# Reciprocals on VectorE as a Newton step on a ScalarE guess, with logarithms and exponentials in groups

## The chip, the cores and the metric

The kernel runs on one core of one Trainium2 chip. The metric is device time in microseconds (us) of that core; less is better.

## What is computed

Three stages in float32: a linear attention with a complex, data-dependent decay, then two feed-forward layers.

```
mag = sqrt(a_re**2 + a_im**2)
scale = minimum(mag, 0.999) / (mag + 1e-6);  a = a * scale        # per channel and token
for t in range(768):                       # S is complex, 48 x 48 per head
    S = a[t][:, None] * S + outer(k[t], v[t])
    y[t] = q[t] @ real(S)
h = y @ w_in                               # 3072 tokens, 384 -> 2048
x = (max(h, 0) + alpha * min(h, 0)) @ w_out
out = x + gate * relu(x @ w1[e]) @ w2[e]   # only tokens with x @ w_skip > 0; e = argmax(x @ w_gate)
```

Batch 4, 8 heads, 768 tokens, head size 48. The division by mag + 1e-6 is one of the two reciprocals of this document. The other comes from the way in which the recurrence is computed: a chunk of 128 tokens is done with matmuls, for which q is multiplied by the product F of the chunk's gates up to its token, and k by 1/F, that is by the conjugate of F over |F|**2. The kernel needs 1/|F|**2 for that.

## The kernel before, in words

Phase 1 works in eight halves of 384 tokens (3 chunks of 128) and runs three things beside each other. A step (`step(h, mlp_too, more)`, written once for each engine) does attention for half h, the first feed-forward layer for half h-1, and prepares the gates of half h+1. The first call (step 0) has no feed-forward layer, the last (step 7) has no next gates, and a last feed-forward layer follows alone. Six of the eight steps are in a loop of three rounds with two steps each. Phase 2 (the experts) comes after and isn't touched.

The order of every engine's work is written out by hand. Between the attention parts stand the blocks of the feed-forward layer, `of_mlp(f)`, f from 0 to 15, with a tail to 18 on TensorE and 16 on the others. For a block f TensorE computes h into `mlp_ps` (L513); ScalarE makes `bent`, a scaled relu of it (L652); VectorE joins it with h to `g` (L907, "the fused operation of f"); ScalarE copies the high part of g of the block before (L658, "high"); VectorE subtracts it to get the low part (L912, "low"); and TensorE uses the parts of block f-3 for the output (L523). `mlp_ps` has two buffers, so TensorE's block f waits for VectorE's fused operation of f-2.

The gates of the next half are prepared by these parts, per chunk of 384 columns:

- `square_gates` (ScalarE, L603), `sum_gates` (VectorE, L770), `root_gates` (ScalarE, L607), `pad_gates` (ScalarE, L613, adds 1e-6), `scale_gates` (VectorE: reciprocal L778, fused minimum and product L780, product L784);
- `within`, `across` and `carry` (VectorE): the running complex products of the gates in a chunk;
- `square_products` and `take_factors` (ScalarE, L626 and L622), `sum_products` (VectorE, L840), `inverse` (VectorE, reciprocal L847), `decay_qk` (VectorE: k times the inverse, L856, then q and k times F, L862).

`decay_qk(nxt, 0)` stands at the end of a step, `decay_qk(h, 1)` and `(h, 2)` in the middle of the next. SyncE's queue is in order too: after `decay_qk(nxt, 0)` it issues the ten moves of q and k to the layout of the heads (`move_qk`, L348), at the end of the step the stores of the finished rows (L380, L381), and at the start of the next the loads of the following half's gates (`load_gates`, L316). TensorE's `scores` of a chunk wait for its moves. `low_y` (L877) and `next_state` (L889 to L901) take a chunk's results out of PSUM on VectorE, `high_y` (L647) does on ScalarE, and `mask_scores` (L870) masks the scores of a chunk on VectorE.

```
sp.wait_ge(qk_made, made)                                 # move_qk: ten moves follow
sp.wait_ge(x2_taken, val(n.n * NC + 2 * NC))              # store_x2: two stores follow
pe.wait_ge(g_made, val(n.n * NF + f + 1))                 # up(n, f), g_made starts at 2
pe.wait_ge(g_lo, val(n.n * NF + f + 4))                   # down(n, f), g_lo starts at 3
act.wait_ge(g_made, val(n.n * NF + f + 3))                # high_g(n, f)
```

## Time and profile before

| | |
|---|---|
| median of 3 runs | 1044.0 us (1043.59 to 1044.29) |
| the profiled execution | 1042.54 us, its span 1040.8 us |
| granted TensorE clock, mean | 0.883 |
| TensorE busy (matmuls) | 765.3 us, 74% of the span |
| VectorE (DVE) busy | 731.2 us, 70% |
| ScalarE (ACT) busy | 320.6 us, 31% |
| GpSimd (POOL) busy | 106.9 us, 10% |
| reciprocals of `scale_gates`, L778 | 24, 61.1 us |
| reciprocals of `inverse`, L847 | 24, 60.0 us |
| phase 1 | to about 813.5 us |

The profile lists one execution. Busy time is the time in which an engine works on an instruction; L778 is line 778 of the kernel before. A share over the whole span mixes stages with different limits, so the prediction reads stretches of it. TensorE's granted clock is given as a share of full speed: its two levels are 1.2 and 2.4 GHz, and a mean between them is a mix.

### The profile page before, as it was taken

To read this page: it belongs to the slowest core of one execution; us is meant where nothing else is said; L and a number is where in the kernel's file an instruction comes from. 1 tells how busy PE (TensorE), PEld (TensorE's weight loads), DVE (VectorE), ACT (ScalarE), POOL (GpSimd) and SP (SyncE) were. 2 spreads that over 40 slices of the span, in tenths; PEclk is the share of its full clock that TensorE was granted. 3 is DMA by queue.
4 is the path that set the end of the run, shared out by engine and by line. 5 is a ranking of instruction groups with operands and counts; after the bars stand their busy time and mean duration, and the time that the engine had idled before them with its cause. 6 is when DMAs were issued, how large, how long until landed. Compare 5 with 4: busy or idle time off the path is not lost. (4 is left out here: it accounts for less than half of the span.)

```text
span 1040.8 us, 16040 instructions
## 1 busy us (share of the span) xinstructions
PE 765.3 (74%) x5430; PEld 735.9 (71%) x5431; DVE 731.2 (70%) x1328; ACT 320.6 (31%) x613; POOL 106.9 (10%) x94
## 2 busy tenths in 40 slices
PE   1514529987896888789689778979999300989897
PEld 1514428877896888689588778869999200989896
DVE  6997988997997899799789979976433410343343
ACT  5532114334232423423242342233333210232321
POOL 4610000000000000000000000000000064232232
PEclk9998668997997898899889989989999755899899
DMA  6633324215233421523342152333210591144440
GB/s 191 211 92 90 101 55 139 53 45 160 66 83 92 121 65 46 164 64 81 94 127 58 45 168 58 82 95 93 61 52 1 211 319 9 34 149 143 146 149 16
DMA packets 87585, 104.82 MB, mean 101 GB/s; under 512 B 21142, under 2 KB 73536, under 8 KB 87488
## 3 DMA queue, kind: packets, MB, share of 16 engines
q1 hardware_dynamic: 84928, 99.76, 32.8%
q0 software_dynamic: 2560, 3.78, 1.2%
q8 instruction: 60, 0.98, 0.4%
q14 instruction: 37, 0.30, 0.1%
HBM read 61.07 MB, written 12.25 MB: 70 GB/s over the span
## 5 line engine op out<-in xcount | busy, mean ns | idle before, releaser
L523 PE MATMUL out_ps<-w_out_hi,g_parts 128*128 128x394 f32 x768 | 235.7, 365 | 36.8 <-DVE g_parts L912 36.8
L513 PE MATMUL mlp_ps<-xT,w_in_hi 128*128 128x384 f32 x768 | 218.0, 367 | 16.7 <-DMA xT<-y_parts 8.1
L523 PEld LDWEIGHTS out_ps<-w_out_hi,g_parts 128*128 128x128 f32 x768 | 154.1, 204 | 42.0 <-DVE g_parts L912 42.0
L513 PEld LDWEIGHTS mlp_ps<-xT,w_in_hi 128*128 128x128 f32 x768 | 147.9, 205 | 21.7 <-issue 12.4
L523 PE MATMUL out_ps<-w_out_lo,g_parts 128*128 128x394 f32 x384 | 138.9, 362 | 0.0
L652 ACT ACTIVATE bent<-mlp_ps,bend_size 128x384 f32<-128x384 f32 x128 | 74.3, 580 | 207.3 <-PE mlp_ps L513 207.1
L513 PE MATMUL mlp_ps<-xT,w_in_lo 128*128 128x384 f32 x384 | 136.6, 356 | 0.0
L907 DVE SCALAR_TENSOR_TENSOR g<-mlp_ps,slope_side,bent 128x384 f32<-128x384 f32 x128 | 78.6, 615 | 79.6 <-ACT bent L652 69.9
L459 PE MATMUL att_ps<-kq 112*128 112x128 f32 x384 | 54.7, 302 | 58.4 <-DMA kq<-qk_dec 58.4
L459 PEld LDWEIGHTS att_ps<-kq 112*128 112x128 f32 x384 | 52.2, 215 | 61.0 <-DMA kq<-qk_dec 47.8
L1250 PE MATMUL mlp_ps<-xT_e,w_sb 128*128 128x128 f32 x624 | 82.3, 297 | 13.1 <-issue 11.5
L1250 PEld LDWEIGHTS mlp_ps<-xT_e,w_sb 128*128 128x128 f32 x624 | 80.5, 212 | 15.6 <-issue 14.2
L658 ACT ACTIVATE g_parts<-g 128x384 fp32r<-128x384 f32 x128 | 66.4, 518 | 59.3 <-DVE g L907 57.1
L523 PEld LDWEIGHTS out_ps<-w_out_lo,g_parts 128*128 128x128 f32 x384 | 78.5, 204 | 0.0
L513 PEld LDWEIGHTS mlp_ps<-xT,w_in_lo 128*128 128x128 f32 x384 | 78.5, 204 | 0.0
L1504 POOL IOTA e_index_i<- 128x8 int32 x1 | 0.1, 134 | 758.5 <-POOLq L135 758.5
L912 DVE TENSOR_TENSOR g_parts<-g,g_parts 128x384 fp32r<-128x384 f32 x128 | 70.1, 548 | 0.3
L1467 DVE SCALAR_TENSOR_TENSOR hT<-mlp_ps,hT 128x256 fp32r<-128x256 f32 x52 | 22.0, 424 | 68.9 <-ACT hT L1322 65.5
L778 DVE RECIPROCAL sq<-sq 128x384 f32<-128x384 f32 x24 | 61.1, 2544 | 1.3 <-ACT sq L613 1.3
L467 PE MATMUL att_ps<-ident,kq 112*128 112x112 f32 x192 | 30.8, 295 | 40.8 <-DVE probs L870 40.8
L847 DVE RECIPROCAL inv<-norms 128x384 f32<-128x384 f32 x24 | 60.0, 2527 | 0.0
L1264 PE MATMUL out_ps<-w_hi,hT 128*128 128x384 f32 x208 | 56.1, 340 | 0.0
(138 smaller groups left out, 1116.2 us busy)
## 6 DMA issues: line engine op xcount, KB each, us to landing
kq<-qk_dec SPq DMA_DIRECT2D x96, 144.0 KB, 3.1
w_sb<-in_w SPq DMA_DIRECT2D x8, 1536.0 KB, 7.3
w_raw<-in_w SPq DMA_DIRECT2D x8, 1536.0 KB, 11.8
gates<-in_a SPq DMA_DIRECT2D x24, 384.0 KB, 5.1
qk_raw<-in_qk SPq DMA_DIRECT2D x24, 384.0 KB, 3.2
xT<-y_parts SPq DMA_DIRECT2D x48, 144.0 KB, 2.8
v_nat<-in_v SPq DMA_DIRECT2D x24, 192.0 KB, 3.1
out<-x SPq DMA_DIRECT2D x8, 576.0 KB, 3.1
```

The source lines that it names most:

```text
L459: last = pe.matmul(ps[:, n * CH:(n + 1) * CH], kq[:, slot, 1, :], kq[:, slot, 0, :], start=True, stop=True)
L467: last = pe.transpose(ps[:, n * ROWS:(n + 1) * ROWS], kq[:, PAIRS * half + n, 1, :], ident[0:ROWS, 0:ROWS])
L513: last = pe.matmul(ps[:, 0:HT], w_in_v[s][:, kk, f * P:(f + 1) * P], xT[n.p][:, kk, m, :], start=(kk == 0 and j == 0), stop=(kk == KT - 1 ...
L523: last = pe.matmul(out_ps[i][:, 0:DL], g_parts[:, f % 4, s, i * P:(i + 1) * P], w_out_v[m][:, f, :], start=(f == 0 and j == 0), stop=(f == ...
L652: act.activation(bent[:, f % 2, :], mlp_ps[f % 2][:, 0:HT], ACT.Relu, scale=bend_size[:, f:f + 1]).then_inc(bent_made, 1)
L658: act.activation(g_parts[:, f % 4, 0, :], g[:, f % 3, :], ACT.Copy).then_inc(g_hi, 1)
L778: dve.reciprocal(s1, s0).then_inc(norm_inv, 1)
L847: dve.reciprocal(of_chunk(inv[:, :], c), of_chunk(norms[:, :], c)).then_inc(f_inverted, 1)
L907: dve.scalar_tensor_tensor(out=g[:, f % 3, :], in0=mlp_ps[f % 2][:, 0:HT], scalar=slope_side[:, f:f + 1], in1=bent[:, f % 2, :], op0=ALU.m ...
L912: dve.tensor_tensor(g_parts[:, f % 4, 1, :], g[:, f % 3, :], g_parts[:, f % 4, 0, :].bitcast(F32), ALU.subtract).then_inc(g_lo, 1)
L1250: last = pe.matmul(mlp_ps[g % 2][:, (f % 2) * P:(f % 2 + 1) * P], w1_v[p][:, kk, f * P:(f + 1) * P], xT[:, kk, :], start=(kk == 0), stop=( ...
L1264: last = pe.matmul(out_ps[0][:, 0:DM], hT[:, a, f, :], w2_v[p][b][:, f, :], start=(f == 0 and j == 0), stop=(f == NFE - 1 and j == 2))
```

## The change

A table-driven guess and one Newton step take the place of both reciprocals. For x = mag + 1e-6 ScalarE computes the guess r = exp(-ln(x)); VectorE computes (x*r - 2) * (min(mag, 0.999)*r), which is the negative of the wanted scale, and a factor -1 in the last product turns the sign back. For x = |F|**2 the guess is exp(-ln(x * 2**63) + 63 ln 2), VectorE computes (x*r - 2)*r, and the product with k has the factor -1.

On ScalarE `pad_gates` is gone; `log_gates` and `guess_gates` come for the norms, `log_inverse` and `guess_inverse` for the products. The logarithms of the three chunks are together, and then the exponentials. On VectorE `scale_gates` has four fused operations and no reciprocal, `inverse` a product and a fused operation. The orders of VectorE and ScalarE are changed around them: the norms are used one f later, `across` and `carry` come somewhat earlier, and `inverse` and `decay_qk` of chunk 0 come behind `of_mlp(16)`. The new semaphores and the second constant column (`shift`) are left out here.

```diff
--- before.py
+++ after.py
...
@@ -606,12 +612,33 @@
                 act.wait_ge(norm_sum, val(chunk_no(h, c) + 1))
                 act.activation(of_chunk(norms[:, :], c), of_chunk(norms[:, :], c), ACT.Sqrt).then_inc(norm_root, 1)
 
-            def pad_gates(h, c):
+            def log_gates(h, c):
 
                 g_ = chunk_no(h, c)
+                s0 = of_chunk(sq[:, 0, :], c)
                 act.wait_ge(norm_root, val(g_ + 1))
-                act.activation(of_chunk(sq[:, 0, :], c), of_chunk(norms[:, :], c), ACT.Identity,
-                               bias=tiny[:, 0:1]).then_inc(norm_eps, 1)
+                act.activation(s0, of_chunk(norms[:, :], c), ACT.Ln, bias=tiny[:, 0:1]).then_inc(norm_log, 1)
+
+            def guess_gates(h, c):
+
+                g_ = chunk_no(h, c)
+                s0 = of_chunk(sq[:, 0, :], c)
+                act.wait_ge(norm_log, val(g_ + 1))
+                act.activation(s0, s0, ACT.Exp, scale=-1.0).then_inc(norm_guess, 1)
+
+            def log_inverse(h, c):
+
+                g_ = chunk_no(h, c)
+                s0 = of_chunk(sq[:, 0, :], c)
+                act.wait_ge(f_summed, val(g_ + 1))
+                act.activation(s0, of_chunk(norms[:, :], c), ACT.Ln, scale=2.0 ** 63).then_inc(f_log, 1)
+
+            def guess_inverse(h, c):
+
+                g_ = chunk_no(h, c)
+                s0 = of_chunk(sq[:, 0, :], c)
+                act.wait_ge(f_log, val(g_ + 1))
+                act.activation(s0, s0, ACT.Exp, bias=shift[:, 0:1], scale=-1.0).then_inc(f_guess, 1)
 
             def take_factors(h):
 
...
@@ -690,14 +717,17 @@
                 if more:
                     root_gates(nxt, 1)
                     root_gates(nxt, 2)
-                    pad_gates(nxt, 0)
+                    log_gates(nxt, 0)
+                    log_gates(nxt, 1)
                 of_mlp(2)
                 high_y(h, 0)
                 if more:
-                    pad_gates(nxt, 1)
+                    log_gates(nxt, 2)
+                    guess_gates(nxt, 0)
                 of_mlp(3)
                 if more:
-                    pad_gates(nxt, 2)
+                    guess_gates(nxt, 1)
+                    guess_gates(nxt, 2)
                 of_mlp(4, 5, 6)
                 back_k(h, 1)
                 of_mlp(7)
...
@@ -706,13 +736,21 @@
                 back_k(h, 2)
                 of_mlp(12)
                 high_y(h, 2)
-                of_mlp(13, 14)
+                of_mlp(13)
                 if more:
                     square_products(nxt, 0)
                     square_products(nxt, 1)
+                    square_products(nxt, 2)
                     take_factors(nxt)
-                    square_products(nxt, 2)
-                of_mlp(15, 16)
+                of_mlp(14)
+                if more:
+                    for c in range(NC):
+                        log_inverse(nxt, c)
+                of_mlp(15)
+                if more:
+                    for c in range(NC):
+                        guess_inverse(nxt, c)
+                of_mlp(16)
                 if mlp_too:
                     take_x2(n)
 
...
@@ -734,10 +772,12 @@
                 square_gates(Half(0, 0), c)
             for c in range(NC):
                 root_gates(Half(0, 0), c)
-            act.wait_ge(bias_made, 1)
+            act.wait_ge(bias_made, 2)
             act.wait_ge(alpha_made, 5)
             for c in range(NC):
-                pad_gates(Half(0, 0), c)
+                log_gates(Half(0, 0), c)
+            for c in range(NC):
+                guess_gates(Half(0, 0), c)
             for kind, n in WEIGHT_ORDER:
                 if kind == "in":
                     split_w_in(n)
...
@@ -746,6 +786,10 @@
             for c in range(NC):
                 square_products(Half(0, 0), c)
             take_factors(Half(0, 0))
+            for c in range(NC):
+                log_inverse(Half(0, 0), c)
+            for c in range(NC):
+                guess_inverse(Half(0, 0), c)
             act.wait_ge(wo_lo, NF)
             step(Half(0, 0), False, True)
             with act.Fori(0, 3) as i:
...
@@ -774,14 +818,18 @@
 
                 g_ = chunk_no(h, c)
                 s0, s1, size = of_chunk(sq[:, 0, :], c), of_chunk(sq[:, 1, :], c), of_chunk(norms[:, :], c)
-                dve.wait_ge(norm_eps, val(g_ + 1))
-                dve.reciprocal(s1, s0).then_inc(norm_inv, 1)
-                dve.wait_ge(norm_inv, val(g_ + 1))
-                dve.scalar_tensor_tensor(out=s0, in0=size, scalar=0.999, in1=s1, op0=ALU.min,
+                dve.wait_ge(norm_guess, val(g_ + 1))
+                dve.scalar_tensor_tensor(out=s1, in0=size, scalar=1e-6, in1=s0, op0=ALU.add,
+                                         op1=ALU.mult).then_inc(norm_step, 1)
+                dve.scalar_tensor_tensor(out=s0, in0=size, scalar=0.999, in1=s0, op0=ALU.min,
+                                         op1=ALU.mult).then_inc(norm_step, 1)
+                dve.wait_ge(norm_step, val(g_ * 2 + 2))
+                dve.scalar_tensor_tensor(out=s1, in0=s1, scalar=2.0, in1=s0, op0=ALU.subtract,
                                          op1=ALU.mult).then_inc(norm_scale, 1)
                 dve.wait_ge(norm_scale, val(g_ + 1))
                 at = of_chunk(gates[h.p][:, :, :], c)
-                dve.tensor_tensor(at, at, s0.unsqueeze(1).broadcast_to([P, 2, DM]), ALU.mult).then_inc(a_normed, 1)
+                dve.scalar_tensor_tensor(out=at, in0=at, scalar=-1.0, in1=s1.unsqueeze(1).broadcast_to([P, 2, DM]),
+                                         op0=ALU.mult, op1=ALU.mult).then_inc(a_normed, 1)
 
             def multiply(h, done, x, y_re, y_im, new_re, new_im, prod_a, prod_b):
 
...
@@ -843,8 +891,12 @@
             def inverse(h, c):
 
                 g_ = chunk_no(h, c)
-                dve.wait_ge(f_summed, val(g_ + 1))
-                dve.reciprocal(of_chunk(inv[:, :], c), of_chunk(norms[:, :], c)).then_inc(f_inverted, 1)
+                s0, s1 = of_chunk(sq[:, 0, :], c), of_chunk(sq[:, 1, :], c)
+                dve.wait_ge(f_guess, val(g_ + 1))
+                dve.tensor_tensor(s1, of_chunk(norms[:, :], c), s0, ALU.mult).then_inc(f_step, 1)
+                dve.wait_ge(f_step, val(g_ + 1))
+                dve.scalar_tensor_tensor(out=of_chunk(inv[:, :], c), in0=s1, scalar=2.0, in1=s0, op0=ALU.subtract,
+                                         op1=ALU.mult).then_inc(f_inverted, 1)
 
             def decay_qk(h, c):
 
...
@@ -853,7 +905,8 @@
                 dve.wait_ge(qk_loaded[m], loads)
                 dve.wait_ge(f_inverted, val(g_ + 1))
                 k_ = qk_raw[:, m, :, 1, :]
-                dve.tensor_tensor(k_, k_, tiles(of_chunk(inv[:, :], c)), ALU.mult).then_inc(k_scaled, 1)
+                dve.scalar_tensor_tensor(out=k_, in0=k_, scalar=-1.0, in1=tiles(of_chunk(inv[:, :], c)), op0=ALU.mult,
+                                         op1=ALU.mult).then_inc(k_scaled, 1)
                 if back(h, c):
                     dve.wait_ge(qk_moved, val(g_ * (32 * len(OP_MOVES))))
                 dve.wait_ge(k_scaled, val(g_ + 1))
...
@@ -935,15 +988,14 @@
                     sum_gates(nxt, 2)
                 decay_qk(h, 1)
                 of_mlp(2)
-                if more:
-                    scale_gates(nxt, 0)
                 low_y(h, 0)
                 next_state(h, 0)
                 of_mlp(3)
                 if more:
+                    scale_gates(nxt, 0)
+                of_mlp(4)
+                if more:
                     scale_gates(nxt, 1)
-                of_mlp(4)
-                if more:
                     scale_gates(nxt, 2)
                 of_mlp(5)
                 mask_scores(h, 1)
...
@@ -965,40 +1017,37 @@
                 if more:
                     within(nxt, 6)
                     within(nxt, 7)
+                    across(nxt, 0)
                 of_mlp(10)
-                if more:
-                    across(nxt, 0)
                 mask_scores(h, 2)
                 if more:
                     across(nxt, 1)
+                    across(nxt, 2)
                 of_mlp(11)
                 if more:
-                    across(nxt, 2)
                     across(nxt, 3)
+                    carry(nxt, 0)
                 of_mlp(12)
                 if more:
-                    carry(nxt, 0)
+                    carry(nxt, 1)
+                    carry(nxt, 2)
                 low_y(h, 2)
                 next_state(h, 2)
                 of_mlp(13)
-                if more:
-                    carry(nxt, 1)
-                    carry(nxt, 2)
                 of_mlp(14)
                 if more:
-                    sum_products(nxt, 0)
-                    sum_products(nxt, 1)
+                    for c in range(NC):
+                        sum_products(nxt, c)
                 of_mlp(15)
+                of_mlp(16)
                 if more:
                     inverse(nxt, 0)
                     decay_qk(nxt, 0)
-                of_mlp(16)
-                if more:
-                    sum_products(nxt, 2)
                     inverse(nxt, 1)
                     inverse(nxt, 2)
 
             dve.memset(tiny[:, :], 1e-6).then_inc(bias_made, 1)
+            dve.memset(shift[:, :], 63.0 * math.log(2.0)).then_inc(bias_made, 1)
             first_h = Half(0, 0)
             for c in range(NC):
                 sum_gates(first_h, c)
```

How it moves instructions, as the built programs have them. First ScalarE at the start of a step in the loop, from the last square of the gates to the first padding and the block f=2; before:

```order
L603 ACTIVATE sq<-gates 128x2x384
L606 REGISTER_ALU
L607 ACTIVATE norms<-norms 128x384
L630 ISA
L596 REGISTER_ALU
L633 ACTIVATE k_back<-att_ps 128x448
```

The same place in the changed program, where a load of ScalarE's table stands between the square and the root:

```order
L609 ACTIVATE sq<-gates 128x2x384
L612 REGISTER_ALU
L613 ACT_TABLE_LOAD
L613 ACTIVATE norms<-norms 128x384
L657 ISA
L602 REGISTER_ALU
L660 ACTIVATE k_back<-att_ps 128x448
```

Some rows on, from the last root to the block f=3 (bent of f=2, high of f=1, high_y, bent of f=3), in the changed program:

```order
L613 ACTIVATE norms<-norms 128x384
L620 ACT_TABLE_LOAD
L620 ACTIVATE sq<-norms,tiny 128x384 x2
L679 ACTIVATE bent<-mlp_ps,bend_size 128x384
L683 REGISTER_ALU
L685 ACTIVATE g_parts<-g 128x384
L670 ISA
L674 ACTIVATE y_parts<-att_ps 112x4x128
L620 ACTIVATE sq<-norms,tiny 128x384
L627 ACT_TABLE_LOAD
L627 ACTIVATE sq<-sq 128x384
L679 ACTIVATE bent<-mlp_ps,bend_size 128x384
```

Before, one padding stood between the last root and bent of f=2, and no load anywhere in the loop. Now there are a load and two logarithms, and a load and an exponential ahead of bent of f=3.

Then VectorE at the end of a step in the loop, from the fused operation of f=15 on; before:

```order
L907 SCALAR_TENSOR_TENSOR g<-mlp_ps,slope_side,bent 128x384
L912 TENSOR_TENSOR g_parts<-g,g_parts 128x384
L847 RECIPROCAL inv<-norms 128x384
L853 REGISTER_ALU
L856 TENSOR_TENSOR qk_raw<-qk_raw,inv 128x3x128
L858 REGISTER_ALU
L862 TENSOR_TENSOR qk_dec<-qk_raw,gates 128x768 x2
L912 TENSOR_TENSOR g_parts<-g,g_parts 128x384
L840 TENSOR_TENSOR norms<-sq 128x384
L847 RECIPROCAL inv<-norms 128x384 x2
```

In the changed program, from the same operation:

```order
L960 SCALAR_TENSOR_TENSOR g<-mlp_ps,slope_side,bent 128x384
L965 TENSOR_TENSOR g_parts<-g,g_parts 128x384 x2
L896 TENSOR_TENSOR sq<-norms,sq 128x384
L898 SCALAR_TENSOR_TENSOR inv<-sq 128x384
L905 REGISTER_ALU
L908 SCALAR_TENSOR_TENSOR qk_raw<-qk_raw,inv 128x3x128
L911 REGISTER_ALU
L915 TENSOR_TENSOR qk_dec<-qk_raw,gates 128x768 x2
```

The low part of f=15 (the second L965) now stands ahead of the inverse and the scaling of chunk 0. On ScalarE the piece that it waits for, from the squares of the products to the high part of f=15, is now:

```order
L679 ACTIVATE bent<-mlp_ps,bend_size 128x384
L683 REGISTER_ALU
L685 ACTIVATE g_parts<-g 128x384
L634 ACT_TABLE_LOAD
L634 ACTIVATE sq<-norms 128x384 x3
L679 ACTIVATE bent<-mlp_ps,bend_size 128x384
L683 REGISTER_ALU
L685 ACTIVATE g_parts<-g 128x384
L641 ACT_TABLE_LOAD
L641 ACTIVATE sq<-sq,shift 128x384 x3
L683 REGISTER_ALU
L685 ACTIVATE g_parts<-g 128x384
```

Before, the three ACTIVATE of L658 and the two of L652 stood there without anything between.

## Rows read from the trace of the kernel before

**Rows 1.** Busy time by stretch: us, TensorE, its weight loads, DVE, ACT, POOL, clock, DMA.

```profile
328.50:420.50 92.00, 77.99 (x554) 75.16 (x555) 78.89 (x146) 30.25 (x60) 0.00 (x0) 0.87 0.32 90
...
693.60:762.50 68.90, 68.22 (x554) 66.89 (x553) 35.93 (x63) 22.21 (x47) 0.00 (x0) 0.99 0.33 88
762.50:813.50 51.00, 50.95 (x288) 50.51 (x286) 17.41 (x32) 17.50 (x39) 0.00 (x0) 1.00 0.07 24
```

**Rows 2.** Groups by line, DVE: busy us, mean ns, idle before them.

```profile
L778 DVE RECIPROCAL sq<-sq 128x384 f32<-128x384 f32 x24 | 61.1, 2544 | 1.3 <-ACT sq L613 1.3
L847 DVE RECIPROCAL inv<-norms 128x384 f32<-128x384 f32 x24 | 60.0, 2527 | 0.0
```

**Rows 3.** DVE's timeline in two steps: start, us, instruction, idle before it.

```profile
340.29 0.56 DVE L770 TENSOR_TENSOR norms<-sq 128x384 f32<-128x384 f32 x1 [3.40 <-ACT sq L603]
...
347.90 2.54 DVE L778 RECIPROCAL sq<-sq 128x384 f32<-128x384 f32 x1
350.48 0.56 DVE L780 SCALAR_TENSOR_TENSOR sq<-norms,sq 128x384 f32<-128x384 f32 x1
351.07 0.96 DVE L784 TENSOR_TENSOR gates<-gates,sq 128x768 f32<-128x768 f32 x1
351.95 0.68 DVE L877 TENSOR_TENSOR y_parts<-att_ps,y_parts 112x512 fp32r<-112x512 f32 x1
...
402.08 0.61 DVE L907 SCALAR_TENSOR_TENSOR g<-mlp_ps,slope_side,bent 128x384 f32<-128x384 f32 x1
...
408.83 0.62 DVE L907 SCALAR_TENSOR_TENSOR g<-mlp_ps,slope_side,bent 128x384 f32<-128x384 f32 x1 [0.54 <-DVE gates L835]
...
415.56 1.83 DVE L862 TENSOR_TENSOR qk_dec<-qk_raw,gates 128x768 f32<-128x768 f32 x2
...
431.14 0.56 DVE L770 TENSOR_TENSOR norms<-sq 128x384 f32<-128x384 f32 x1 [4.90 <-ACT sq L603]
...
436.81 0.62 DVE L907 SCALAR_TENSOR_TENSOR g<-mlp_ps,slope_side,bent 128x384 f32<-128x384 f32 x1
```

**Rows 4.** SyncE's queue at the turn of a step.

```profile
417.46 6.22 SPq L348 DMA_DIRECT2D kq<-qk_dec  x10
...
425.13 2.94 SPq L316 DMA_DIRECT2D gates<-in_a  x3
```

**Rows 5.** ACT's timeline at the start of the kernel.

```profile
7.55 0.84 ACT L603 ACTIVATE sq<-gates 128x768 f32<-128x768 f32 x1 [1.13 <-DMA gates<-in_a]
8.41 1.28 ACT L607 ACT_TABLE_LOAD   x1
9.70 1.35 ACT L607 ACTIVATE norms<-norms 128x384 f32<-128x384 f32 x3
```

**Rows 6.** ACT's timeline at the head of a step in the loop.

```profile
432.86 0.84 ACT L603 ACTIVATE sq<-gates 128x768 f32<-128x768 f32 x1 [0.71 <-DMA gates<-in_a]
433.61 0.51 ACT L607 ACTIVATE norms<-norms 128x384 f32<-128x384 f32 x1
...
435.69 0.61 ACT L613 ACTIVATE sq<-norms,tiny 128x384 f32<-128x384 f32 x1
436.20 0.58 ACT L652 ACTIVATE bent<-mlp_ps,bend_size 128x384 f32<-128x384 f32 x1
...
439.62 0.58 ACT L652 ACTIVATE bent<-mlp_ps,bend_size 128x384 f32<-128x384 f32 x1 [1.30 <-PE mlp_ps L513]
```

**Rows 7.** ACT's timeline behind the last carry of the prologue: the three squares.

```profile
67.47 2.31 ACT L626 ACTIVATE sq<-gates 128x768 f32<-128x768 f32 x3 [6.63 <-DVE gates L835]
```

**Rows 8.** TensorE's timeline: scores at the start of steps 4 and 1, matmuls at low clock.

```profile
425.12 2.05 PE L459 MATMUL att_ps<-kq 112*128 112x128 f32 x16 [0.61 <-DMA kq<-qk_dec]
...
433.86 0.84 PE L513 MATMUL mlp_ps<-xT,w_in_hi 128*128 128x384 f32 x2
434.50 0.52 PE L513 MATMUL mlp_ps<-xT,w_in_lo 128*128 128x384 f32 x1
434.82 0.84 PE L513 MATMUL mlp_ps<-xT,w_in_hi 128*128 128x384 f32 x2
...
155.04 3.78 PE L459 MATMUL att_ps<-kq 112*128 112x128 f32 x16 [11.58 <-DMA kq<-qk_dec]
```

More of the change, by code:

```diff
@@ L1 @@
+import math
 from contextlib import ExitStack
@@ L150, in phase1 @@
         tiny = sb("tiny", [P, 1])
+        shift = sb("shift", [P, 1])
         gates = [sb(f"gates{i}", [P, 2, NC * DM]) for i in range(2)]
@@ L217, in phase1 @@
         norm_root = sem("norm_root")
-        norm_eps = sem("norm_eps")
-        norm_inv = sem("norm_inv")
+        norm_log = sem("norm_log")
+        norm_guess = sem("norm_guess")
+        norm_step = sem("norm_step")
         norm_scale = sem("norm_scale")
@@ L224, in phase1 @@
         f_summed = sem("f_summed")
+        f_log = sem("f_log")
+        f_guess = sem("f_guess")
+        f_step = sem("f_step")
         f_inverted = sem("f_inverted")
@@ L943, in step @@
                 if more:
-                    scale_gates(nxt, 1)
+                    scale_gates(nxt, 0)
                 of_mlp(4)
                 if more:
+                    scale_gates(nxt, 1)
                     scale_gates(nxt, 2)
```

## The prediction

> **What bounds the kernel now.** I read the time by stage first [rows 1]. The last MLP alone (51.0 us) and the step before it, which prepares no gates (68.9 us), keep TensorE busy for 99% at a granted clock of 0.99 to 1.00. A step that also prepares the next half's gates takes about 91 us; there TensorE is busy for 78 us of 92 and VectorE for 79. So the gates' work costs some 23 us a step, and TensorE has room: VectorE, in its fixed order, sets the pace of six steps. In the groups by line [rows 2] the two reciprocals are the dearest things that it does for the gates: 2.54 and 2.53 us each, 24 of each, 121 us in all; an ordinary sum or fused operation of the same 384 columns takes 0.56 us [rows 3].
>
> VectorE's timeline shows where a step turns round [rows 3]. Let S be the start of the first gate sum and D the end of the scaling of q and k for the next half's chunk 0. S is 340.29 and D 417.39 (77.1 us); the next S is 431.14 (13.75 us later). Between S and D VectorE hardly waits. Between D and S it waits 4.90 us for ScalarE's square, and that for the gates' transfer. SyncE's queue says why [rows 4]: its ten moves of q and k take from 417.46 to 423.68, then come two stores, then the gates' loads at 425.13, on which the square ahead of S waits. So **the period is S to D on VectorE, plus 13.75 us of transfers that start with D**. Whatever VectorE does after D is hidden under those transfers.
>
> ScalarE is busy for only 30 of 92 us [rows 1], but it stands in VectorE's way at two places: bent, which VectorE's fused operation of a block needs, and the high part, which its low part needs, are ScalarE's, and it too works in order.
>
> **The change part by part.**
>
> *Scaling of the gates (VectorE, before D).* Removed: one reciprocal, 2.58 us from its start to the next instruction's in [rows 3]. Added: two operations of the kind of L780. By its spacing of 0.59 us in [rows 3], 0.53 for the one that nothing waits for, and 0.06 more for the final product in its new form, it is 4.05 us before and about 2.73 after. Saving 1.32 us a chunk, **4.0 us a step**. Bounds: nothing lost on the new form (4.3) and 0.15 us lost on every new operation (3.1).
>
> *Inverses.* A reciprocal of 2.55 becomes a product and a fused operation, 0.55 + 0.62 with a little between, 1.22 us. Three times a step, but only chunk 0 lies before D: the other two come after it, where 4.90 us of waiting hide them. So **1.4 us**, not 4.1.
>
> *ScalarE at the head of the step.* The order listing shows a table load before the roots, before the first logarithms and before the exponentials; before the change the loop has none. The one load in the middle of the work [rows 5] takes 1.28 us, and the activation behind it starts at once (8.41, 9.70). Between the last square (to 433.70) and bent of f=2 ScalarE does one root, two copies, two roots and one padding [rows 6]; now there are two loads and a second logarithm more: 2 x 1.28 + 0.51, and 0.2 for overlaps lost. VectorE reaches the fused operation of f=2 at 436.81 [rows 3] and bent ends at 436.77 [rows 6]: there is no slack at all, so all of it is a stall, **+3.3 us**. Behind it the new order helps: low_y and next_state (3.0 us) come first, and meanwhile ScalarE does high_y, the third logarithm, the exponentials' load and the first guess, 0.60 + 0.51 + 1.28 + 0.45, then bent of f=3. That ends some 0.2 us before VectorE wants it. TensorE loses nothing there: it was done with its part of f=3 at 439.6 [rows 6], some 4 us before the new order asks for it.
>
> *The middle.* Same operations; the multiplication of k in the fused form costs perhaps 0.07 us each, twice, **+0.1**. The carries for chunks 1 and 2 (5.2 us: from 402.08 and 1.0 for block 13 to 0.54 before 408.83) move ahead of low_y of chunk 2. TensorE's matmuls of block 15 wait for the fused operation of block 13, so TensorE will stand idle ahead of them and do them at its low clock: nine at 0.32 us [rows 8], 2.9 us.
>
> *The tail, up to D.* Before [rows 3]: fused 13 at 402.08, two carries of 5.2 us, fused 14 at 408.83, two sums, fused 15, inverse, scaling to 417.39: 15.3 us. After, counted from the new fused 13 and with the carries already done: the squares (2.31 us, [rows 7]) run under low_y and next_state. fused 13, low 12, fused 14, low 13 to 2.0; sums to 3.5. ScalarE: high 13 to 1.15, load to 2.43, logarithms to 4.06 (the last needs the third sum, 3.5), bent 15 to 4.6 (TensorE has finished its block 15 at 3.6). VectorE waits **1.15 us** for that; fused 15 and low 14 to 5.6. ScalarE: high 14 to 5.0, load to 6.3, three exponentials at 0.50 to 7.9, high 15 to 8.3. VectorE's low 15, now ahead of the inverse, waits for high 15: **2.75 us**. Then low 15 to 8.8, inverse to 10.05, scaling to 12.6. With the 5.2 us of carries that is 17.8 against 15.3: **+2.5 us** (the two waits 3.9, low 15 and a third sum moved ahead of D 1.0, gaps of 0.9 gone, the saving of 1.4 in the inverse counted).
>
> *After D.* The ten moves of q and k, the stores and the gates' loads follow D as now; TensorE is done with the last block earlier than before. It will stand idle for some 5 us before the scores of chunk 0, where it now waits 0.61 us [rows 8], and start them at the lower of its two clocks: 16 matmuls took 3.78 us after an idle of 11.58 us and 2.05 us here [rows 8]. In a step with gates that is covered, for S comes 13.75 us after D and the scores end 11.6 after it.
>
> Sum for a step: -4.0 + 3.3 + 0.1 + 2.5 = **+1.9 us**, six times: +11.4.
>
> *Prologue and step 0.* At the start two more loads, two logarithms and one exponential precede the first scaling (+4.1 us) against the 4.0 us that it saves; POOL's work, which now meets fewer reciprocals, may add 1 us. Behind the last carry nothing covers the squares, and the two chains of load, three activations, load, one activation (2.4 us of squares, then 4.9) stand in place of one reciprocal: D comes 3.2 us later. In step 0 the stall at low_y is 1.5 and the scaling saves 4.0; the end of the step loses 3.2 more but has low_y and next_state (3.0) beside the chain. Together **+2.6 us** at the D of step 0.
>
> *Last attention step.* TensorE bounds it [rows 1], so the slow scores and about 1.5 us of slow matmuls behind them are paid in full: **+3.0 us**. The expert stage isn't touched.
>
> Total 11.4 + 2.6 + 3.0 = +17.0 us on the profiled execution, whose own time is 1042.5 (span 1040.8). The median of the three runs shown, 1044.0, is 1.5 above it. So **1061 us**.
>
> **A page against the rows.** In [rows 5] a square ends at 8.39, the load runs from 8.41 to 9.69 and the root begins at 9.70: a switch costs 1.3 us and nothing beside. The Trainium skill, page "ScalarE: Activation LUTs", section "What ACT_TABLE_LOAD costs", has the same 1283 ns for the load but adds a drain of about 1380 ns at each switch. By that page the four loads that VectorE waits for would add some 5.4 us a step, and the sum would be about 1098. The same page, section "Table sets: the hidden batching unit", says that one set holds both logarithm and exponential, so that one load would do for the two; the order listing, which has one before each, does not bear that out.
>
> **The rivals.**
> 1. *The waits don't appear* (faster). Place: VectorE's fused operation of f=2 and low 15. If ScalarE were ahead of VectorE at both, a step would change by 1.9 - 3.3 - 3.9 = -5.3 us, less what low_y then waits for, say -5.0: six of them and nothing at the ends give 1044 - 30 = 1014. It decides from the point where the two waits of 7.2 us together fall under 5.3. For it: ScalarE is idle for two thirds of a step. Against it: at 436.77 and 436.81 there is no slack. Chance 0.11.
> 2. *Break-even.* The waits come out a quarter smaller and the ends cost nothing: 1044 give or take 2. Chance 0.05.
> 3. *TensorE's clock.* Idle stretches of 4 us at blocks 13 to 15 and 5 us ahead of the scores keep it low for longer; if matmuls at the low clock make bent 15 or mask of chunk 0 late by 1.5 us in each step, it is 1061 + 9 to 12, about 1072. For it: the granted clock is 0.87 in such a step already [rows 1]. Against it: 0.4 us of slack at block 15 and 2 us at the mask. Chance 0.12.
> 4. *A pause at each switch*, as long as the load: 1.28 us for each of four loads on the chain less 0.2 hidden under the sums, 4.9 a step, 29 in six, 7 at the ends: 1097. Against it: [rows 5]. The page named above would give this. Chance 0.04.
>
> The forecast has 0.68.
>
> **How the numbers follow.** A change of 0.2% (2 us) is about what a measurement of this kernel can tell. The forecast's own bounds: scaling saves 3.1 to 4.3, and the two waits 6.2 to 8.2 us, so +0.6 to +3.8 us a step; with 3 to 7 us at the ends that is 1051 to 1074. With 2 in 10 left out, of which the fast rival takes one and the pause and some of the third the other, the range is 1047 to 1074. Faster by over 0.2%: 0.11. Within 0.2%: 0.05. Slower by over 0.2%: 0.84.
>
> **What would show it.** VectorE's busy time falls by some 60 us (121 of reciprocals out, about 60 in) and the time does not follow. ScalarE has some 40 table loads of 1.28 us, against three. VectorE waits about 3.3 us a step for bent at f=2, about 1.1 for bent at f=15 and 2.75 for high 15; D to the next S stays near 13.8 to 15, and S to D goes from 77 to 79. TensorE waits about 5 us for kq at the head of each step. I am wrong if VectorE reaches f=2 later than 3 us behind the last sum (then the head is no stall), or if D to S shrinks, for then the transfers were not what held the step's turn.

## The result, and the profile after

| | before | after |
|---|---|---|
| median | 1044.14 us (4 runs, 1043.59 to 1044.83) | 1056.08 us (4 runs, 1055.94 to 1056.94) |
| the profiled execution | 1042.54, span 1040.8 | 1056.21, span 1054.5 |
| VectorE busy | 731.2 us | 664.7 us |
| ScalarE busy | 320.6 us | 404.4 us |
| table loads on ScalarE | 3 | 41 |

The changed kernel takes 1.0116 times as long (95% interval 1.0098 to 1.0133): 1.2% slower, though VectorE, which sets the pace of six steps, works 66.5 us less. Busy time by stretch in the changed kernel, with the columns of [rows 1]: a step with gates, the step without, the last feed-forward layer.

```profile
337.50:429.50 92.00, 76.14 (x555) 72.55 (x554) 71.11 (x153) 41.75 (x76) 0.00 (x0) 0.89 0.30 89
705.60:777.40 71.80, 67.37 (x536) 66.36 (x537) 33.37 (x61) 19.35 (x40) 0.00 (x0) 0.95 0.29 84
777.40:828.40 51.00, 50.94 (x288) 50.50 (x286) 17.42 (x32) 17.51 (x39) 0.00 (x0) 1.00 0.06 24
```

In such a stretch VectorE has gone from 78.9 to 71.1 us of 92 and TensorE from 78.0 to 76.1: both idle more. Only ScalarE is busier, 41.8 us where it had 30.3. The groups by line (busy us, mean ns, idle before them) say what came in place of the reciprocals of [rows 2]:

```profile
L822 DVE SCALAR_TENSOR_TENSOR sq<-norms,sq 128x384 f32<-128x384 f32 x24 | 17.5, 731 | 4.9 <-ACT sq L627 4.9
L898 DVE SCALAR_TENSOR_TENSOR inv<-sq 128x384 f32<-128x384 f32 x24 | 13.4, 558 | 0.8
L960 DVE SCALAR_TENSOR_TENSOR g<-mlp_ps,slope_side,bent 128x384 f32<-128x384 f32 x128 | 78.4, 615 | 94.3 <-ACT bent L679 84.6
L613 ACT ACT_TABLE_LOAD x8 | 10.3, 1283 | 0.1
...
L641 ACT ACT_TABLE_LOAD x8 | 10.3, 1283 | 0.1
```

Of these loads there are five groups of eight (L613, L620, L627, L634 and L641, all with the same numbers): five switches of ScalarE's table in each of eight rounds (the prologue and steps 0 to 6), 51 us; the loop before had none. The idle of 0.1 us in front of them says that ScalarE goes into each load at once.

VectorE's timeline shows where they are felt. First the head of a step (it starts at S, the first L814), then the end of the same step (D, 518.52, is the end of the last row). The columns are those of [rows 3].

```profile
440.16 0.56 DVE L814 TENSOR_TENSOR norms<-sq 128x384 f32<-128x384 f32 x1 [9.83 <-ACT sq L609]
...
444.48 1.83 DVE L915 TENSOR_TENSOR qk_dec<-qk_raw,gates 128x768 f32<-128x768 f32 x2
449.77 0.62 DVE L960 SCALAR_TENSOR_TENSOR g<-mlp_ps,slope_side,bent 128x384 f32<-128x384 f32 x1 [3.47 <-ACT bent L679]
...
454.72 0.55 DVE L822 SCALAR_TENSOR_TENSOR sq<-norms,sq 128x384 f32<-128x384 f32 x1
...
457.24 0.61 DVE L960 SCALAR_TENSOR_TENSOR g<-mlp_ps,slope_side,bent 128x384 f32<-128x384 f32 x1
...
505.96 0.61 DVE L960 SCALAR_TENSOR_TENSOR g<-mlp_ps,slope_side,bent 128x384 f32<-128x384 f32 x1
...
510.52 0.62 DVE L960 SCALAR_TENSOR_TENSOR g<-mlp_ps,slope_side,bent 128x384 f32<-128x384 f32 x1 [1.09 <-ACT bent L679]
511.06 0.55 DVE L965 TENSOR_TENSOR g_parts<-g,g_parts 128x384 fp32r<-128x384 f32 x1
514.29 0.56 DVE L965 TENSOR_TENSOR g_parts<-g,g_parts 128x384 fp32r<-128x384 f32 x1 [2.69 <-ACT g_parts L685]
...
516.69 1.83 DVE L915 TENSOR_TENSOR qk_dec<-qk_raw,gates 128x768 f32<-128x768 f32 x2
```

Three waits for ScalarE on the way from S to D stand there, 3.47, 1.09 and 2.69 us. ScalarE's timeline in the same two places says what it did meanwhile:

```profile
442.47 0.84 ACT L609 ACTIVATE sq<-gates 128x768 f32<-128x768 f32 x1 [1.31 <-DMA gates<-in_a]
443.33 1.28 ACT L613 ACT_TABLE_LOAD   x1
444.63 0.52 ACT L613 ACTIVATE norms<-norms 128x384 f32<-128x384 f32 x1
445.06 0.96 ACT L660 ACTIVATE k_back<-att_ps 128x448 f32<-128x448 f32 x2
445.90 0.93 ACT L613 ACTIVATE norms<-norms 128x384 f32<-128x384 f32 x2
446.86 1.28 ACT L620 ACT_TABLE_LOAD   x1
448.15 1.12 ACT L620 ACTIVATE sq<-norms,tiny 128x384 f32<-128x384 f32 x2
449.18 0.56 ACT L679 ACTIVATE bent<-mlp_ps,bend_size 128x384 f32<-128x384 f32 x1
...
510.92 1.28 ACT L641 ACT_TABLE_LOAD   x1
512.22 1.63 ACT L641 ACTIVATE sq<-sq,shift 128x384 f32<-128x384 f32 x3
513.75 0.51 ACT L685 ACTIVATE g_parts<-g 128x384 fp32r<-128x384 f32 x1
```

From the square to bent of f=2 ScalarE never pauses: it is idle over half of the step, and still late by the two loads and two logarithms that stand ahead of the one piece that VectorE needs.

### The profile page after: what moved, and what is told of

Its sections match the earlier page's. It is cut to its first block and busy times, and to the rows that moved or that the text cites. A ratio compares the mean times of both kernels' runs of the same rounds, so it can differ in the third digit from the quotient of the medians.

```text
span 1054.5 us, 16210 instructions
## 1 busy us (share of the span) xinstructions
PE 763.5 (72%) x5430; PEld 734.5 (70%) x5431; DVE 664.7 (63%) x1377; ACT 404.4 (38%) x723; POOL 109.6 (10%) x94
## 3 DMA queue, kind: packets, MB, share of 16 engines
q0 software_dynamic: 2560, 3.78, 1.2%
## 5 line engine op out<-in xcount | busy, mean ns | idle before, releaser
L529 PE MATMUL out_ps<-w_out_hi,g_parts 128*128 128x394 f32 x768 | 221.1, 347 | 0.2 <-DVE g_parts L965 0.2
L529 PEld LDWEIGHTS out_ps<-w_out_hi,g_parts 128*128 128x128 f32 x768 | 146.2, 193 | 0.5 <-DVE g_parts L965 0.5
L529 PE MATMUL out_ps<-w_out_lo,g_parts 128*128 128x394 f32 x384 | 133.2, 347 | 0.0
L465 PE MATMUL att_ps<-kq 112*128 112x128 f32 x384 | 65.4, 341 | 91.8 <-DMA kq<-qk_dec 91.8
L465 PEld LDWEIGHTS att_ps<-kq 112*128 112x128 f32 x384 | 61.6, 249 | 96.0 <-DMA kq<-qk_dec 78.1
L1299 PEld LDWEIGHTS mlp_ps<-xT_e,w_sb 128*128 128x128 f32 x624 | 80.1, 212 | 15.1 <-issue 15.1
L965 DVE TENSOR_TENSOR g_parts<-g,g_parts 128x384 fp32r<-128x384 f32 x128 | 70.3, 549 | 16.6 <-ACT g_parts L685 16.1
L529 PEld LDWEIGHTS out_ps<-w_out_lo,g_parts 128*128 128x128 f32 x384 | 74.1, 193 | 0.0
L1371 ACT ACTIVATE hT<-mlp_ps 128x256 fp32r<-128x256 f32 x52 | 19.9, 384 | 98.3 <-PE mlp_ps L1299 98.3
L814 DVE TENSOR_TENSOR norms<-sq 128x384 f32<-128x384 f32 x24 | 13.2, 555 | 66.6 <-ACT sq L609 66.6
```

The lines of the kernel that those rows point to most:

```text
L465: last = pe.matmul(ps[:, n * CH:(n + 1) * CH], kq[:, slot, 1, :], kq[:, slot, 0, :], start=True, stop=True)
L529: last = pe.matmul(out_ps[i][:, 0:DL], g_parts[:, f % 4, s, i * P:(i + 1) * P], w_out_v[m][:, f, :], start=(f == 0 and j == 0), stop=(f == ...
L965: dve.tensor_tensor(g_parts[:, f % 4, 1, :], g[:, f % 3, :], g_parts[:, f % 4, 0, :].bitcast(F32), ALU.subtract).then_inc(g_lo, 1)
L1299: last = pe.matmul(mlp_ps[g % 2][:, (f % 2) * P:(f % 2 + 1) * P], w1_v[p][:, kk, f * P:(f + 1) * P], xT[:, kk, :], start=(kk == 0), stop=( ...
```

## The experiments

All are compared with the kernel before in the same session. Each is also read by its own trace: in steps 1 to 5 of the loop, S to D is the length of VectorE's part, D to the next S the length of the turn (both worked out from the rows of the gate sum and of the scaling of q and k). Before, S to D is 76.2 to 77.1 us (mean 76.5) and the turn 13.8 to 15.1; in the changed kernel 77.4 to 79.2 (mean 78.3) and 13.6 to 15.3. So the turn did not move, and the change sits between S and D.

### Does the time hang on what stands ahead of D?

The prediction's frame is that a step lasts S to D on VectorE, plus a fixed turn. Two kernels put one more reciprocal into each step of the kernel before, writing to a tile that nothing reads: the same 2.5 us of work, once ahead of D (chunk 0) and once behind it (chunk 2).

```diff
                 dve.wait_ge(f_summed, val(g_ + 1))
+                if c == 0:      # e_after_d: c == 2
+                    dve.reciprocal(scratch[:, :], of_chunk(norms[:, :], c))
                 dve.reciprocal(of_chunk(inv[:, :], c), of_chunk(norms[:, :], c)).then_inc(f_inverted, 1)
```

Expected of the one ahead of D:

> The same extra reciprocal in every inverse of chunk 0, ahead of D. Chain theory: S to D is 79.6 and D to S stays 13.8 to 15; 8 x 2.5 = 20 us more, 1063. Rival, the step is bound by TensorE's last blocks and the stores behind them (which also wait for it here, but would have slack): under 10 us more.

Expected of the one behind it:

> The kernel before with one reciprocal more in every inverse of chunk 2 (its result goes to a tile that nothing reads), which lies behind D. Chain theory: 2.5 us a step disappear under the transfers, S to S is unchanged in six steps, and only step 0 and the prologue may pay: 1044 to 1048. Rival, VectorE's busy time counts: 8 x 2.5 = 20 us more, 1064.

Ahead of D: 1065.8 us against 1044.4, ratio 1.0209 (1.0183 to 1.0234), S to D 78.7 to 79.4. Behind it: 1046.2, ratio 1.0020 (1.0003 to 1.0037), S to D unchanged at 76.1 to 76.7. The same instruction costs 21 us or 2 us, by its place alone. VectorE's timeline of the kernel with the reciprocal behind D:

```profile
414.43 1.83 DVE L865 TENSOR_TENSOR qk_dec<-qk_raw,gates 128x768 f32<-128x768 f32 x2
...
419.57 2.49 DVE L849 RECIPROCAL scratch<-norms 128x384 f32<-128x384 f32 x1
...
430.73 0.56 DVE L771 TENSOR_TENSOR norms<-sq 128x384 f32<-128x384 f32 x1 [4.67 <-ACT sq L604]
```

VectorE still waits 4.67 us ahead of S for the gates. Not quite all of the 2.5 us is hidden: the turn is 13.9 to 16.3 us here, where it was 13.8 to 15.1. This is why the change earned next to nothing for two of its three cheaper inverses.

### Which half of the change costs?

e_head keeps the Newton step for the norms, with its orders, and gives the products' inverse, the carries and the end of the step back to the old code. e_tail does the reverse. Of both, the core against the changed kernel:

```diff
# e_head
 def inverse(h, c):
-    dve.tensor_tensor(s1, of_chunk(norms[:, :], c), s0, ALU.mult).then_inc(f_step, 1)
-    dve.scalar_tensor_tensor(out=of_chunk(inv[:, :], c), in0=s1, scalar=2.0, in1=s0, op0=ALU.subtract,
-                             op1=ALU.mult).then_inc(f_inverted, 1)
+    dve.reciprocal(of_chunk(inv[:, :], c), of_chunk(norms[:, :], c)).then_inc(f_inverted, 1)
# e_tail
 def scale_gates(h, c):
-    dve.scalar_tensor_tensor(out=s1, in0=size, scalar=1e-6, in1=s0, op0=ALU.add, op1=ALU.mult).then_inc(norm_step, 1)
...
+    dve.reciprocal(s1, s0).then_inc(norm_inv, 1)
```

> Only the scaling of the gates has the Newton step (logarithm and exponential, norms one f later); inverse and the end of the step are as before the change, with reciprocals. Chain theory (time is VectorE's S to D plus a fixed D to S; table loads stand on that chain): the scaling gives back 4.6 us a step and the stall ahead of the fused operation of f=2 costs 3.5, so S to D is about 76 us and the whole 1044 + 3 for the prologue - 2 for step 0 - 7 = about 1038. Rival, the loss is in the new order of the end of the step and the loads cost nothing: 4.6 us a step for seven, about 1012 to 1015.

> Only the inverse and the end of the step are changed; the scaling keeps padding and reciprocal. Chain theory: the end of the step costs 2.4 us, and the load for the roots, which the loop now needs, 1.3 more ahead of f=2: S to D near 80.8, total 1044 + 22 + 6 for prologue and step 0 + 2 for the last step = about 1074. Rival, busy time counts (VectorE does 4 us less a step): about 1015 to 1040.

e_head: 1038.8 us against 1042.9, ratio 0.9948 (0.9924 to 0.9971), S to D 75.2 to 75.6. e_tail: 1071.5, ratio 1.0264 (1.0233 to 1.0294), S to D 80.3 to 80.8. So one half gains 0.5% and the other loses 2.6%. To see where, the places of VectorE's fused operations of f=2, 5 and 13 and of D, in us from S, in step 4 (worked out from the rows of each timeline):

| | S at | f=2 | f=5 | f=13 | D |
|---|---|---|---|---|---|
| before | 431.14 | 5.67 | 23.74 | 60.86 | 76.17 |
| after | 440.16 | 9.61 | 23.12 | 65.80 | 78.36 |
| e_head | 426.65 | 9.54 | 23.05 | 60.12 | 75.43 |
| e_tail | 444.89 | 7.56 | 25.65 | 67.95 | 80.48 |

At f=2 the changed kernel is 3.9 us late (3.47 of the stall, the rest a longer wait for the gates' transfer ahead of the third sum), by f=5 it is 0.6 early: the cheaper scaling pays the stall back and little more. From f=5 to D it loses 2.8. In e_tail f=2 is late as well, by 1.9 us, though its norms are done as before. ScalarE's timeline there shows 1.28 us of it:

```profile
447.94 1.28 ACT L612 ACT_TABLE_LOAD   x1
449.23 0.53 ACT L612 ACTIVATE norms<-norms 128x384 f32<-128x384 f32 x1
```

The exponentials at the end of a step leave their table in, so the roots at the next head must load theirs. In e_head the exponentials of the head do the same, and the load is there too. Either half alone pays for that load, the whole pays once. This makes the halves add up: -1.2 (e_head, mean 75.3 against 76.5) and +4.1 (e_tail, 80.6), less the 1.28 counted twice, is +1.6; measured +1.8 from 76.5 to 78.3.

### Are the switches the cost?

e_joint changes nothing but which table the logarithms load: one that serves exponentials too. Two loads a step are left, 17 in all. e_noswitch needs none in the loop: it also writes the root as exp(0.5 ln s) and the guess as exp(-0.5 ln s), where s is the squared norm. It leaves the 1e-6 out of the guess, and keeps it in the Newton step.

```diff
# e_joint
+                if c == 0:
+                    act.preload_act_table_set("natural_log_exp_and_others")
                 act.wait_ge(norm_root, val(g_ + 1))
                 act.activation(s0, of_chunk(norms[:, :], c), ACT.Ln, bias=tiny[:, 0:1]).then_inc(norm_log, 1)
# e_noswitch (the set is loaded once, ahead of the first square)
-    act.activation(of_chunk(norms[:, :], c), of_chunk(norms[:, :], c), ACT.Sqrt).then_inc(norm_root, 1)
+    act.activation(of_chunk(norms[:, :], c), of_chunk(norms[:, :], c), ACT.Ln).then_inc(norm_root, 1)
-    act.activation(s0, of_chunk(norms[:, :], c), ACT.Ln, bias=tiny[:, 0:1]).then_inc(norm_log, 1)
+    act.activation(s0, of_chunk(norms[:, :], c), ACT.Exp, scale=-0.5).then_inc(norm_log, 1)
-    act.activation(s0, s0, ACT.Exp, scale=-1.0).then_inc(norm_guess, 1)
+    act.activation(of_chunk(norms[:, :], c), of_chunk(norms[:, :], c), ACT.Exp, scale=0.5).then_inc(norm_guess, 1)
```

> The change, but one load ahead of the first logarithm of a step brings the set with both logarithm and exponential: two loads a step where it has five. Chain theory: the load at f=3 had slack and the one ahead of the logarithms of the inverse nearly so, only the one ahead of the last exponentials counts: S to D 1.3 us shorter than the changed kernel's 78.3, and some 4 us at the ends, about 1044. Rival, the order of the end and not the loads costs the time: 1056 as the changed kernel.

> As the change, but norm and guess both come as exponentials of half the logarithm of the squared norm, out of the set with both functions: no load after the first. (1e-6 is added in the Newton step alone.) Chain theory: two loads less ahead of f=2 (2.6 us) and one ahead of high 15 (1.3): S to D about 74.4, six steps give 23.5 and the ends some 7, about 1025. Rival, the order or the added activations cost the time: 1050 to 1056.

e_joint: 1042.8 us, ratio 0.9990 (0.9972 to 1.0008): two lines take back the whole loss, and no more. S to D is 76.2 to 77.3. e_noswitch: 1023.6, ratio 0.9794 (0.9763 to 0.9826), S to D 73.7 to 74.6. The same two waits in VectorE's timeline, first of e_joint:

```profile
439.24 0.62 DVE L962 SCALAR_TENSOR_TENSOR g<-mlp_ps,slope_side,bent 128x384 f32<-128x384 f32 x1 [3.47 <-ACT bent L681]
...
499.96 0.62 DVE L962 SCALAR_TENSOR_TENSOR g<-mlp_ps,slope_side,bent 128x384 f32<-128x384 f32 x1 [1.06 <-ACT bent L681]
...
502.30 0.56 DVE L967 TENSOR_TENSOR g_parts<-g,g_parts 128x384 fp32r<-128x384 f32 x1 [1.26 <-ACT g_parts L687]
```

and of e_noswitch:

```profile
425.19 0.62 DVE L961 SCALAR_TENSOR_TENSOR g<-mlp_ps,slope_side,bent 128x384 f32<-128x384 f32 x1 [0.43 <-ACT bent L679]
...
486.11 0.62 DVE L961 SCALAR_TENSOR_TENSOR g<-mlp_ps,slope_side,bent 128x384 f32<-128x384 f32 x1 [1.09 <-ACT bent L679]
...
488.45 0.56 DVE L966 TENSOR_TENSOR g_parts<-g,g_parts 128x384 fp32r<-128x384 f32 x1 [1.26 <-ACT g_parts L685]
```

The wait of low 15 falls from 2.69 to 1.26 in both, by one load and the gap around it. The stall at f=2 stays in e_joint, whose two loads of the head are the same, and falls by 3.04 in e_noswitch. Taking out both gives 3.04 + 1.43 = 4.5 us a step; S to D fell by 4.1 from its mean of 78.3. The wait of 1.1 for bent 15 is no matter of loads: it stays without them. With the tail's loads gone ScalarE reaches the third logarithm sooner, but that needs VectorE's third sum, and bent 15 stands behind it.

### Can the Newton step win by more?

v_one_set takes e_noswitch and reorders what is left for the chain to D: only what chunk 0 needs stands ahead of D, the inverse and the scaling of q and k move before f=15, and chunks 1 and 2 go behind D. At the head the logarithms move behind bent of f=2, and the scaling of chunk 0 stands ahead of low_y again. What each of these moves is worth was not tried alone. The diff shows the end of the step:

```diff
 # ScalarE, tail
                 of_mlp(14)
                 if more:
-                    for c in range(NC):
-                        log_inverse(nxt, c)
+                    log_inverse(nxt, 0)
+                    guess_inverse(nxt, 0)
                 of_mlp(15)
...
 # VectorE, tail
+                if more:
+                    sum_products(nxt, 0)
                 of_mlp(13)
                 of_mlp(14)
                 if more:
-                    for c in range(NC):
-                        sum_products(nxt, c)
+                    inverse(nxt, 0)
+                    decay_qk(nxt, 0)
                 of_mlp(15)
                 of_mlp(16)
                 if more:
-                    inverse(nxt, 0)
-                    decay_qk(nxt, 0)
+                    sum_products(nxt, 1)
+                    sum_products(nxt, 2)
                     inverse(nxt, 1)
```

> The kernel without switches, and with the orders fitted to the chain: guesses one by one where each is wanted, no logarithm ahead of bent of f=2, scaling of chunk 0 ahead of low_y again; at the end the sum of chunk 0 first, its logarithm and exponential behind high 13, inverse and scaling of chunk 0 ahead of the fused operation of f=15, the other two chunks behind low 15. Chain theory: S to D about 68.5 to 70, six times 7 to 8.5 us less than the kernel before, and some 8 less at the ends: 985 to 1000. Rival, TensorE becomes the bound (68.9 us a step, and idle at its head): S to S stays above 87, 1015 or more.

1002.5 us, ratio 0.9593 (0.9571 to 0.9616). S to D is 68.4 to 69.1, as expected; the total is 2.5 us above the range that was expected, since the turn grew to 15.3 to 16.9 us. SyncE's queue in this kernel, around a D at 306.31:

```profile
304.07 3.69 SPq L360 DMA_DIRECT2D f_pair<-f_packed  x6
308.00 7.60 SPq L354 DMA_DIRECT2D kq<-qk_dec  x10
```

The ten moves of q and k begin 1.7 us after D. In [rows 4] they began 0.07 us after it. D has come so early that it meets the six transfers of the last factors in the queue. v_queue issues these at the head of the next step; e_queue makes the same edit in the kernel before.

```diff
                         load_qkv(h, c + 1)
+                        if mlp_too and c == 0:
+                            move_factors(h)
                         move_qk(h, c + 1)
...
                 if more:
-                    move_factors(h.plus(1))
                     move_qk(h.plus(1), 0)
```

> v_one_set with the six transfers of the last factors (move_factors) issued at the head of the next step, behind the loads of the gates, and not ahead of the ten moves of q and k. In v_one_set the ten moves began 1.7 us after D (308.00 against 306.31), since SyncE was still issuing the factors' six (304.07, 3.69 us); before and in the changed kernel they began 0.07 us after D. If that is the miss of v_one_set, D to S falls from 15.3 to 16.9 to 13.7 to 15.2, S to D stays 68.4 to 69.1, and six steps give 10 us: 992, between 989 and 996. Rival (the transfers themselves are slower when D comes that early, since they meet those of y, state and factors): D to S stays above 15 and the time above 999.

> The same move of SyncE's six transfers in the kernel before, where D comes long after them. Nothing is late there, so the time stays at that of before within 1 us, S to D 76.2 to 77.1 and D to S 13.7 to 15.1. Rival (the order of SyncE's queue costs something in every kernel): 1034 to 1040.

v_queue: 990.9 us, ratio 0.9478 (0.9455 to 0.9501), the fastest version here. e_queue: 1043.3, ratio 0.9992 (0.9976 to 1.0008), the turn 13.8 to 15.7 us. SyncE's queue in v_queue, where D is at 301.76:

```profile
301.84 7.21 SPq L354 DMA_DIRECT2D kq<-qk_dec  x10
309.27 1.11 SPq L386 DMA_DIRECT2D out<-x  x1
...
311.74 2.57 SPq L322 DMA_DIRECT2D gates<-in_a  x3
...
315.77 3.77 SPq L360 DMA_DIRECT2D f_pair<-f_packed  x6
```

In three of five turns D to S is back at 13.5 to 13.7. In the other two, every second step of the loop, it is 15.8 and 16.6, against 15.0 and 15.1 before. The ten moves are not what is new there: in the same two turns of the kernel before they already take 7.49 and 7.15 us to issue, not the 6.22 of [rows 4], and the gates' three loads are issued 12.2 us behind D in both, against 12.6 and 11.9 here. But from there to S pass 4.1 and 3.9 us, where it was 2.8 and 3.0. Why the gates come later was not tried.

## Why the prediction was right

The forecast was 1061 us and 1056.1 came. Of the 4.9 us between them 3.3 are terms of the sum (17.0 us where the profiled executions lie 13.7 apart). The other 1.6 are scatter: the forecast added 1.5 us for a profiled execution below its median, and that of the changed kernel (1056.21) is not below its own. Step by step:

- **The frame held.** D to S stayed at 13.6 to 15.3, and work behind D was nearly free (2 us for a reciprocal there, 21 ahead of it).
- **The stall at f=2: right.** 3.47 us where 3.3 was said. It is the two loads: without them it is 0.43. Counted from S, f=2 comes 3.94 us later in this step and 3.65 on average over the six, since the third sum waits longer for the gates; the sum had no term for that.
- **The tail: right.** From the fused operation of f=13 to D it was to take 12.6 us, and took 518.52 - 505.96 = 12.56. The waits were said to be 1.15 and 2.75 and are 1.09 and 2.69.
- **The scaling: mis-sized.** It was to save 4.0 us a step and saves 4.6: a chunk takes 457.24 - 454.72 = 2.52 us, not 2.73. The term took 0.06 us off for the fused form of the last product. There is no such cost: the new form has a mean of 1072 ns (x24), the old one the same 1072. Another 0.06 is the operation that nothing waits for (0.47 us to the next, not 0.53), and 0.08 is a slip: 4.05 - 2.58 + 0.59 + 0.53 + 0.06 is 2.65, not 2.73. A loop step thus grew by 1.66 us (the D at the end of step 0 is 2.96 later than before, that at the end of step 6 12.91 later: 9.95 over six), not 1.9: 0.6 less by the scaling, 0.35 more at f=2. In step 4, by the table: 0.6 us gained up to f=5, 0.4 lost from there to f=13 beside the moved carries, 2.5 lost in the tail.
- **Prologue and step 0: the sum near, by luck.** 2.6 was said and 2.96 measured, but the terms as written add up to 2.0: a D of the prologue 4.3 us late, and 2.3 won back in step 0. It is 5.6 us late, and 2.6 are won back. The prologue's scaling starts 4.4 us later and saves nothing instead of 4.0, see the last section; the running products then get 3.2 us of that back beside GpSimd. Behind the last carry 2.8 us are lost, where 3.2 was said. Step 0 does not win by its own S, which follows D by 2.0 us instead of 4.8: VectorE then waits 7.04 us for the scores, and the mask of chunk 0 is still 5.4 us late (90.55 against 85.14). The scaling wins it back: the mask of chunk 1 is 2.0 us late (107.79 against 105.78), for 4.6 saved less a wait of 1.2 at low_y. The end of step 0 loses nearly 1 us again.
- **The last attention step: the slow matmuls right, the total too dear.** 3.0 was said, 2.0 measured (the first result row of that step is 14.88 us late, D 12.91). TensorE idles 5.59 us ahead of the scores, where 0.68 stood before, and runs at a granted clock of 0.50 from 710.03 to 716.10, where it had 1.00 from its first score on. From the first score to the end of phase 1 it takes 118.3 us instead of 115.2: that is 3.1, as said. What the sum lacked is that the scores begin 7.6 us behind D instead of 8.7: the ten moves took 6.23 us to issue at this turn, where they took 7.18 before. Why the moves took less was not tried.
- **The expert stage** ended 1.2 us sooner relative to phase 1, where the sum had zero. Nothing of it was changed. From the end of phase 1 to the end of the span pass 226.2 us in the changed kernel, 227.4 in the kernel before and up to 231.3 in the others here, so 1.2 lies within what varies between kernels anyway.

TensorE's timeline, scores at the start of steps 4 and 7 of the changed kernel:

```profile
434.11 3.14 PE L465 MATMUL att_ps<-kq 112*128 112x128 f32 x13 [5.85 <-DMA kq<-qk_dec]
...
710.03 2.29 PE L465 MATMUL att_ps<-kq 112*128 112x128 f32 x9 [5.59 <-DMA kq<-qk_dec]
```

The view's windows end within both groups; all 16 matmuls take 3.78 us in each, where they took 2.05 before ([rows 8], and in step 7 too).

The rivals fell. The waits were there (the first), and the ratio's interval, 1.0098 to 1.0133, leaves no room for a break-even (the second). TensorE's clock did not add 9 us: the granted clock of a step with gates is 0.89, not under the 0.87 of before. A pause at each switch did not show: the square ends at 443.31, the load runs 443.33 to 444.61, and the root begins at 444.63. The Trainium skill, page "ScalarE: Activation LUTs", section "What ACT_TABLE_LOAD costs", has a drain of about 1380 ns beside the load's 1283 ns; the trace agrees with the load alone. What the Trainium skill says on the same page, section "Table sets: the hidden batching unit", that one set serves logarithm and exponential, was set aside in the prediction because the changed program loads one before each. The set exists, as e_joint shows. This program got it only when it asked for it: 41 loads without, 17 with.

## What to carry to other kernels

Replacing a dear operation by cheap ones pays only where it stands on the chain, and a guess on another engine brings that engine's order onto the chain: price the table switches by what is queued behind them (here the five loads a step turned a gain of 19 us, that of e_noswitch, into a loss of 12, though VectorE worked 66 us less in both). When several table functions alternate, look for one set that holds them all, or rewrite the functions so that they share one: here that turned 1.2% slower into 2.1% faster, with the orders fitted to the chain into 4.1%, and with the queue put right into 5.2%. After each gain, read the in-order queue behind the new end of the chain again: what was harmless in it (e_queue, no difference) was worth some 1.2% once D came earlier (0.9593 to 0.9478 of the kernel before).

## What the runs showed of the hardware that was not expected

A reciprocal is not slowed by GpSimd, and an operation with two operands in SBUF is. VectorE's timeline in the prologue of the changed kernel:

```profile
15.94 0.56 DVE L822 SCALAR_TENSOR_TENSOR sq<-norms,sq 128x384 f32<-128x384 f32 x1 [4.91 <-ACT sq L627]
...
18.47 2.71 DVE L822 SCALAR_TENSOR_TENSOR sq<-norms,sq 128x384 f32<-128x384 f32 x1
21.10 2.69 DVE L824 SCALAR_TENSOR_TENSOR sq<-norms,sq 128x384 f32<-128x384 f32 x1
```

and GpSimd's, in the same kernel:

```profile
17.76 5.61 POOL L1117 TENSOR_TENSOR w_in_lo<-gates,w_in_hi 128x1024 fp32r<-128x1024 f32 x2 [14.07 <-ACT w_in_hi L769]
```

The same operation takes 0.56 us alone and 2.71 beside GpSimd. In the kernel before, the reciprocals at 15.64 and at 22.56 take their usual 2.54 us beside GpSimd's subtractions, the first beside the same one (16.84 to 21.82):

```profile
15.64 2.54 DVE L778 RECIPROCAL sq<-sq 128x384 f32<-128x384 f32 x1
...
22.56 2.54 DVE L778 RECIPROCAL sq<-sq 128x384 f32<-128x384 f32 x1
```

```profile
16.84 4.98 POOL L1068 TENSOR_TENSOR w_in_lo<-gates,w_in_hi 128x1024 fp32r<-128x1024 f32 x2 [13.16 <-ACT w_in_hi L731]
```

Per chunk the old form has two operations with both operands in SBUF, the new one four. So the prologue's three scalings took 17.3 us before (11.59 to 28.93) and 19.0 after (15.94 to 34.90): beside GpSimd the Newton form is the dearer one. The Trainium skill, page "SBUF — State Buffer", section "Who interferes with whom", has this rule: an instruction of VectorE with two SBUF inputs contends with a GpSimd instruction that reads SBUF, and one with at most one SBUF input, outside the 2-port modes, does not. The trace agrees, and the wait has the length of the rest of GpSimd's instruction: 18.47 plus the rest of the first subtraction (2.1 us; it ends by half of the 5.61 from 17.76) plus 0.56 gives 21.1, and the operation ended at 21.18.
